# A second weight request one batch later, and a block of zeros stored in the expert stage

## What is computed

```python
scores = 0.125 * x @ state.T ; a = softmax(scores)
xread = a @ state
a2 = softmax(0.125 * state @ x.T)
sread = a2 @ x
x = concatenate([xread, sread], axis=2)       # (8*(512+32), 512) rows

e_idx = argmax(x @ w_gate, axis=1)            # one of 8 experts for each row
ye = relu(x @ w1[e]) @ w2[e]                  # 512 -> 1024 -> 512
x = gate_w * sigmoid(x @ w_output_gate)[e] * ye

h = x @ w_in                                  # 512 -> 2048
g = where(h >= 1, h, where(h <= -1, 0, (h + 1)**2 / 4))
out = g @ w_out                               # 2048 -> 512
```

## Time and profile before

| | |
|---|---|
| median of 3 runs | 1325.91 us (1325.71 to 1326.55) |
| the profiled execution | 1319.86 us |
| its span, first to last instruction | 1318.1 us |
| attention stage | to about 151 us |
| expert stage | about 151 to 572 us |
| dense stage | the rest |
| granted TensorE clock | full in all of the slices of the page |
| busy share of PE / DVE / ACT / POOL | 99% / 72% / 31% / 29% |

### The profile page before, as it was taken

How to read it: one execution, slowest core, us unless ns; L and a number is a source line. 1 busy time by engine, 2 the same in 40 slices (tenths; PEclk the granted TensorE clock), 3 DMA queues, 4 the chain that set the end, 5 groups by cost and what they waited for, 6 DMA issues and landing times.

```text
span 1318.1 us, 20459 instructions
## 1 busy us (share of the span) xinstructions
PE 1304.4 (99%) x6383; PEld 1088.8 (83%) x6384; DVE 953.1 (72%) x2034; ACT 410.7 (31%) x641; POOL 384.5 (29%) x212
## 2 busy tenths in 40 slices
PE   8999999999999999999999999999999999999998
PEld 6999888888888888888888888888888888888887
DVE  4666889999999998957777577675775766757344
ACT  3455422222222222432222222222222222222232
POOL 2377462966690939370010100100101001001010
PEclk9999999999999999999999999999999999999999
DMA  6856545665863647630010100100101001000000
GB/s 153 246 165 186 170 136 135 165 169 143 192 162 108 165 113 226 191 113 17 16 41 16 41 17 16 38 17 8 40 16 40 16 16 40 16 8 33 0 33 17
DMA packets 104447, 113.44 MB, mean 86 GB/s; under 512 B 49104, under 2 KB 68560, under 8 KB 103888
## 3 DMA queue, kind: packets, MB, share of 16 engines
q1 hardware_dynamic: 62864, 64.57, 18.1%
q10 hardware_dynamic: 35072, 30.42, 8.7%
q0 software_dynamic: 6464, 17.86, 3.6%
HBM read 69.80 MB, written 43.02 MB: 86 GB/s over the span
## 4 chain that ended last, share of the span: by engine, by line
PE 96%; DMA 1%; DVE 1%; SPq 1%; ACT 0%; ACTq 0%; issue 0%; POOL 0%; DVEq 0%
PE area L1837 28%; PE area L1851 28%; PE area L1786 16%; PE area L1741 16%; PE area L1554 2%; PE area L1524 2%; PE area L1544 1%; DMA xin<-in_x 1%; SPq L374 1%; PE area L1511 1%; PE area L1571 1%; DMA st_diag<-in_state 0%; PE area L1578 0%; ACTq L374 0%; PE area L1563 0%
## 5 line engine op out<-in xcount | busy, mean ns | idle before, releaser
L1837 PE MATMUL area<-ys,W 128*128 128x512 f32 (+1 forms) x1728 | 394.1, 377 | 0.0
L1851 PE MATMUL area<-W,gs 128*128 128x512 f32 x1632 | 393.5, 389 | 0.0
L1837 PEld LDWEIGHTS area<-ys,W 128*128 128x128 f32 x1728 | 313.3, 188 | 61.1
L1851 PEld LDWEIGHTS area<-W,gs 128*128 128x128 f32 x1632 | 305.3, 188 | 62.9 <-DVE gs L1406 0.2
L1307 DVE STREAM_TRANSPOSE area<-hrow 32x256 f32<-32x256 f32 x576 | 262.6, 456 | 38.6 <-ACT hrow L770 29.9
L845 ACT ACTIVATE gate<-gate,half_col 128x512 f32<-128x512 f32 (+1 forms) x144 | 100.7, 700 | 376.4 <-DVE gate L1396 374.6
L1786 PE MATMUL area<-W,hs 128*128 x888 | 210.3, 392 | 0.0
L1396 DVE TENSOR_SCALAR gate<-area 128x512 f32<-128x512 f32 (+1 forms) x144 | 95.3, 662 | 159.0 <-PE area L1837 158.9
L652 POOL DMA_INDIRECT out<-orow,out_row x32 | 30.8, 963 | 592.5 <-ACT orow L861 504.2
L1741 PE MATMUL area<-W,xs 128*128 x864 | 201.9, 389 | 0.0
L1786 PEld LDWEIGHTS area<-W,hs 128*128 128x128 f32 x888 | 164.9, 188 | 40.4 <-issue 7.9
(11 more groups left out here) (217 smaller groups left out, 805.0 us busy)
## 6 DMA issues: line engine op xcount, KB each, us to landing
stage<-in_moe_w SPq DMA_DIRECT2D x64, 256.0 KB, 4.7
stage<-in_moe_w SPq DMA_DIRECT2D x16, 1024.0 KB, 6.8
sorted_y<-ytile ACTq DMA_DIRECT2D x38, 256.0 KB
tile_y<-ytile ACTq DMA_DIRECT2D x38, 256.0 KB
xtile<-slot_x ACTq DMA_DIRECT2D x144, 64.0 KB, 2.3
yrow<-sorted_y SPq DMA_DIRECT2D x32, 256.0 KB, 2.6
xin<-in_x SPq DMA_DIRECT2D x60, 128.0 KB, 3.0
stage<-in_moe_w_in SPq DMA_DIRECT2D x4, 1024.0 KB, 5.1
```

Source lines behind the costliest of these rows:

```text
L1837: last = nc.tensor.matmul(HIDDEN[n % 2][:, 0:width], wq[:, wp, :], ys[par][:, yp, k, 0:width], start=(k == 0 and wp == HI and yp == HI), s ...
L1851: last = nc.tensor.matmul(SUMS[a], gs[n % 2][:, gp, a * P:(a + 1) * P], W[:, q // 2 + 2, wp, at:at + DM], start=(n == 0 and gp == HI and w ...
```

## The change

Four things are moved, and two small ones are new.

- SP requests only unit 0 of the first expert in step 2; unit 1 is requested in step 3, behind batch 3's eight requests, where the zeros were.
- The zeros are stored by SP behind the four units of expert 1 and ahead of those of expert 2. Their source is `yrow[0]`, a row buffer of the dense stage that nobody uses by then, since `zero` is memory that the expert stage has given to other things. The transfer has the same size and destination.
- New: POOL clears `yrow[0]` (128x512) after it has split expert 1, and signals `yrow_cleared`; SP waits for that in front of the store, and so in front of all of expert 2's units.
- SP's wait for `tails_zeroed` goes from in front of the first two expert tiles to in front of the first loads of the dense stage, ACT's from L794 to behind the loop over the tiles that always exist.

```diff
             for b in range(2, B):
                 load_x_next(b, b % 2)
-                if b == 3:
-                    sp.dma_start(tile_y[TT * P:TILES * P, :].rearrange("(t p) d -> p t d", p=P),
-                                 zero[:, :].unsqueeze(1).to_broadcast([P, TILES - TT, DM])).then_inc(tails_zeroed, 16)
-                if b == 2:
-                    for q in range(2):
-                        expert_unit(0, q)
+                if b in (2, 3):
+                    expert_unit(0, b - 2)
...
-            sp.wait_ge(tails_zeroed, 16)
             for t in range(2):
                 load_rows(sp, t, t * P)
             load_expert(1, range(2))
             load_expert(1, range(2, 4))
+            sp.wait_ge(yrow_cleared, 1)
+            sp.dma_start(tile_y[TT * P:TILES * P, :].rearrange("(t p) d -> p t d", p=P),
+                         yrow[0][:, :].unsqueeze(1).to_broadcast([P, TILES - TT, DM])).then_inc(tails_zeroed, 16)
             with sp.Fori(2, E) as e:
                 load_expert(e, range(4))
...
             sp.wait_ge(y_stored, 32 * (BIG + E + 2 + ST))
+            sp.wait_ge(tails_zeroed, 16)
...
                 if q == 1:
                     scatter_info(1)
+            pool.memset(yrow[0][:, :], 0.0).then_inc(yrow_cleared, 1)
...
-            act.wait_ge(tails_zeroed, 16)
             act.wait_ge(half_up, 1)
...
             with act.Fori(3, TT - 3) as t:
                 turn(t)
+            act.wait_ge(tails_zeroed, 16)
```

More of the change, by code:

```diff
@@ L264, in build @@
         slot_weights_known = sem("slot_weights_known")
+        yrow_cleared = sem("yrow_cleared")
         tails_zeroed = sem("tails_zeroed")
```

## The result

The changed kernel takes 1329.38 us (median of 10 runs, 1327.54 to 1332.3), the kernel before, run beside it, 1325.03 us (10 runs, 1323.47 to 1327.49). The ratio is 1.0037, 95% interval 1.0027 to 1.0048: slower by 0.37%, where 1325.6 us and "no change" were predicted. The time is also above the range's upper end.

What follows compares the result with a forecast made beforehand. PE was taken to bound the kernel, about 4 us winnable, no slack in the expert stage. Step 3 -0.3, step 4 -0.1, store +0.1 summed to -0.3 us: median 1325.6 us, own range 1325.0 to 1326.2, wider range 1323.8 to 1328.5.

Steps and rivals of the forecast that it cites:

- the deadline that it worked out: Expert stage, at turn_x: the tile may be there at 219.6 us without moving anything; what DVE loses beyond, PE loses too.
- The store, +0.1 us, bounds 0 and 2.9: Expert stage: the zeros' store beside a tile of x was expected to cost 0.1 us, bounds 0 and 2.9.
- the row that was called nearest: POOL's scatters beside the zeros took 4.6 us more; added to the tile's 3.3 us, this gave 7.9, nothing lost.
- the upper bound: Expert stage: the tile stands behind the whole store, 13.7 us, plus one transfer of 1.9 us: 2.9 us late.
- The step on SP's new wait: Ahead of expert 2's requests: they go out from about 207.7 us; POOL still gets its units, cost 0, 4 us to spare.
- The rule on turns: DMA engines go round the queues packet by packet, so xtile gets its turn and the 2.9 us would not occur.
- Rival C: Expert stage: the store holds up a tile, 2.9 us, or 8 to 11 behind the weights too; chance 0.20, 0.10 over 2.7 us.
- Unit 1 and the zeros out of the attention stage, -0.4 us: Attention stage: shorter waits for xin, -0.3 us in step 3 and -0.1 in step 4.
- the long request: Batch 3's request of 1.45 us: taken as belonging to SP's instruction list, sliding four requests later; gain 0, bounds 0 and 0.8.
- rival A: Attention stage: the waits for xin in steps 3 and 4 go entirely, 1.49 us, giving 1324.4; chance 0.15.
- One sign of being wrong: The mechanism is wrong if PE waits between 205 and 235 us or attention ends over 1 us earlier or later.
- POOL's memset: After expert 1's split: clearing takes at most 0.84 us, while POOL then stands idle 24.25 us; cost 0.

Runs made afterwards that it cites:

- gap2: Changed kernel with the store behind a landed tile, between expert 2's units 1 and 2, and expert 0's units 0 and 1 both in step 2: 0.9999.
- gap3: Changed kernel with expert 2's units 0 and 1 requested first, then the store once a tile has landed, then units 2 and 3: 0.9997.
- the repeat of after: The changed kernel profiled and timed once more, unaltered, against the kernel before: 1.0033.
- apart: Changed kernel in which SP waits behind the store until the zeros have landed, then requests expert 2's weights: 0.9994.
- double2: Changed kernel with expert 2's units 0 and 1 first, then the store twice, the second when the first has landed, then units 2 and 3: 1.0004.
- rows_after: Changed kernel with a tile of x requested as whole 2048 B rows instead of 512 B pieces; for timing only: 1.0012.
- only_wait: Kernel before with SP requesting expert 2's first weights only after expert 1's last unit is split, zeros still in step 3: 1.0005.
- swapped: Changed kernel with expert 2's first 2 MB requested ahead of the store instead of behind it: 1.0004.
- late_weights: Kernel before with SP waiting, ahead of expert 2's 2 MB, for ACT's copy right in front of a tile's requests; no store there: 0.9994.

## Why the prediction was wrong

**What bounds the kernel, and where a loss can arise: right.** PE had no slack in the expert stage, and the loss is there, at the one place that the prediction named (`turn_x`, then the split of `xs`, then PE), beyond the deadline that it worked out (10.3 us after the request).

**The store, +0.1 us, bounds 0 and 2.9: this is the step that failed.** It should have been +4.7. Three things in it were wrong.

First the row that was called nearest. The scatters beside the zeros came 4.6 us late, and that was carried over to the tile, as "about the same transfer": 3.3 + 4.6 = 7.9 us behind the last request, which is 9.4 behind the first. But the tile is 576 packets, nearly all of 512 B, while POOL's queue moved 0.23 MB in 56 packets beside the zeros (before, 54 to 56 us), some 4 KB each; and behind step 3's zeros there were no weights. Measured: 15.1 us behind the first request.

Second the upper bound, the whole store and one transfer of 1.9 us behind it. It left out what stands behind the store in SP's list. The step on SP's new wait had said that expert 2's eight requests now go out at once behind the store, and charged for it only at POOL, which wants them ("Cost 0, with 4 us to spare"; that was right). The party that pays is not in that chain: it is ACT's queue, which shares the engines with them.

Third the price of a request. While the store is young, ACT's four take 4.0 us instead of the 1.85 of the earlier trace rows, and no packet of the tile passes for 4 to 5 us after the first request, where in the two traces of before it is 1.3 to 2.7. Both belong in T, and both were taken as in before.

In the repeat of after the sum is 4.2 us until the first packets (212.19 to about 216.4) + 8.6 us to 225, in which 161 + 364 = 525 of them pass + 2.2 us for the last ones, the landing and DVE's start at 227.25 = 15.0 us.

**The rule on turns** (the Trainium skill, "DMA: Bandwidth & Descriptors", Queues, rings and completion order) agrees with the packets of two queues, 362 to 364 and 314 to 309. The packet of that page holds several descriptors, and these counts don't show whether a turn is one of the profile's packets or several; they show equal numbers. What was drawn from the rule does not agree: that `xtile` gets its turn, so that nothing happens. With equal numbers, each small packet is paid for with a neighbour's large one. In the first 4 to 5 us after the request there were no turns either, which that rule doesn't lead one to expect.

**Rival C** had the mechanism in its second half: a tile behind the store and the weights too, a landing at about 231 and a loss of 8 to 11 us, at a chance of 0.10. The size was too large: it used 13.7 us for the store and 10.0 for the weights, one behind the other, 24.1 us from the store's issue to the landing. Measured from 208.79 to 227.25 us: 18.5, of which the store took 10.7. It was held to be unlikely by the row of the scatters, the same mis-sized row.

**Unit 1 and the zeros out of the attention stage, -0.4 us: not shown.** gap2 has the zeros out of the attention stage and gap3 has unit 1 moved besides; they are at 0.9999 and 0.9997, each within 0.1% of no change. -0.4 us is 0.03%, below what can be told. Within this step one argument was wrong. SP's eight requests for batch 3 took 5.59 to 6.39 us in all 8 traces in which units 0 and 1 stand in step 2, and 5.33 or 5.34 us in all 9 in which unit 1 is behind them; in after they are at

```profile
48.92 5.33 SPq L375 DMA_DIRECT2D xin<-in_x  x8
```

where the earlier trace rows has 6.08. So the long request did come from the weights and went with them, as in rival A; it did not slide four requests later. But A's price didn't follow. PE's waits for `xin` sum to 1.3 to 3.4 us, 2.1 in the mean, in the six traces with before's attention stage, and to 0.7 to 2.4, 1.6 in the mean, in seven with that of after (the first trace of after puts its own down to "issue"). That is -0.5 us, about the -0.4 of the forecast, from traces that scatter by more. The two traces with both units in step 2 and only the zeros gone have 0.9 and 0.8, so if anything is gained there, it isn't by the move of unit 1. PE's wait for DVE's copies of x, which the prediction named as what is late next, is 0.4 and 1.2 us in the two traces of before and 2.5 and 1.4 in the two of after. So nothing of it can be seen in the time. One sign of being wrong that the prediction named did come up here, an attention stage that ends more than 1 us later: 4.3 us in the first two traces, 1.0 in the repeats. As traces of one kernel differ by 1.4 and 2.0 us there, and the store alone has the whole loss, it can't be told from scatter.

**POOL's memset, both waits for** `tails_zeroed`**, SP's new wait at POOL: cost 0, right.** PE waits for none of them in the expert stage of any trace, and in apart, where expert 2's weights are asked for only at 215 us, the time is before's.

**The chances.** 0.10 for slower by over 0.2% was too little for a case whose two halves (weights at once behind the store, no slack on PE) stood in the text, and whose only counter-argument was one row of another packet size.

## What to carry to other kernels

For a small transfer on the critical path count its packets, and not its bytes alone: packets times the time of one turn beside the neighbour's packets, plus the wait before its first one, and set that against its deadline. For double2 this gives 4.5 + 576 / 155 = 8.2 us, and the tile's last packet had passed by 221.5, 8.3 us after its request. It isn't a full account: for rows_after it gives 3.9 + 192 / 61 = 7.0 us, and the last packet passed after 11.2. When a wait is put in front of requests, look for who shares the DMA engines in the stretch in which they now all go out together, not only for who consumes them. A large store that has no deadline belongs directly behind a landing of the small transfers, or behind the large loads, or with a wait for it in front of them; all three were before's time here, with intervals that end at 1.0013 at the most.

## What was not expected of the hardware

Behind 2 MB of weights or a 2816 KB store, the first packet of a tile came 4 to 5 us after its request in every kernel (only_wait: request at 208.00, none until 213; swapped: 207.75 and 212; rows_after: 207.19 and 211), though the packets then pass in about equal numbers (239 of the tile to 173 in only_wait, 175 to 170 in swapped). Where the weights were requested behind the tile instead (late_weights), the first came within 1.3 us. Larger packets alone didn't bring the tile ahead: in rows_after its 192 packets, 128 of them of 2048 B, took from 211.1 to 218.4 us, where 61 a microsecond would be 3.1 us. By the microsecond from 211 they are 37, 11, 23, 25, 19, 36, 36 and 5, so they come in groups of 48, as many as one request has; why the groups stand apart was not tried.

Requests cost their engine more while a large store is young: ACT's four took 3.6 to 4.2 us instead of 1.85, SP's eight 7.8 to 8.55 instead of 3.9, and ACT's with the store alone too (apart, 4.21). Some 7 us behind the store they took 3.0 and 3.2 (gap3, gap2), and 11.5 us behind it 1.89 (swapped). Why was not tried.
